# The remainder products of w_out's rest columns on 64 weight columns, and a new order inside the last group

## The reference, cut to what matters

```
h = x @ w_in                             # 192 -> 2048
g = h * (1.0 / (1.0 + np.exp(-1.702 * h)))
return (g @ w_out).astype(np.float32)    # 2048 -> 192
```

## Time and profile before

| what | value |
|---|---|
| median of three runs | 1128.98 us |
| time of the profiled execution | 1129.01 us |
| its span, first to last instruction | 1127.2 us |
| TensorE matmul busy | 1113.8 us (99%) |
| TensorE weight load busy | 914.3 us (81%) |
| VectorE busy | 803.6 us (71%) |
| ScalarE busy | 620.5 us (55%) |
| GpSimd busy | 7.9 us (1%) |

### The profile page before, as it was taken

How to read it: one execution, slowest core, us unless ns; L and a number is a source line. 1 busy time by engine, 2 the same in 40 slices (tenths; PEclk the granted TensorE clock), 3 DMA queues, 4 the chain that set the end, 5 groups by cost and what they waited for, 6 DMA issues and landing times.

```text
span 1127.2 us, 21689 instructions
## 1 busy us (share of the span) xinstructions
PE 1113.8 (99%) x9748; PEld 914.3 (81%) x9748; DVE 803.6 (71%) x714; ACT 620.5 (55%) x655; POOL 7.9 (1%) x9
## 2 busy tenths in 40 slices
PE   7999999999999999999999999999999999999998
PEld 4788878888888888888888888888888888888886
DVE  7998988677576866759667596775867757686322
ACT  6676655565554646455464555545556555454543
POOL 2000000000000000000000000000000000000000
PEclk9999999999999999999999999999999999999999
DMA  8601010101001010010100101001010100100000
GB/s 274 218 7 53 15 53 2 39 29 40 29 1 40 29 40 29 1 40 29 40 29 1 65 4 40 29 22 46 1 40 29 40 29 1 40 29 1 29 1 29
DMA packets 8892, 42.68 MB, mean 38 GB/s; under 512 B 1056, under 2 KB 1312, under 8 KB 6496
## 3 DMA queue, kind: packets, MB, share of 16 engines
q1 hardware_dynamic: 8400, 40.51, 10.9%
q0 software_dynamic: 400, 0.79, 0.4%
HBM read 24.77 MB, written 12.58 MB: 33 GB/s over the span
## 4 chain that ended last, share of the span: by engine, by line
PE 94%; DVE 4%; ACT 1%; DMA 0%; issue 0%; ACTq 0%; DVEq 0%; SPq 0%
PE hid L630 45%; PE acc_main L646 30%; PE acc_rest L646 20%; DVE conv L393 1%; DVE gate_lo L548 1%; DVE prod L386 1%; DMA gate<-in_x_first 0%; ACT gate_hi L313 0%; ACT gate L310 0%; DVE hid L469 0%; DVE w L441 0%; DVE prod L411 0%; DVE prod L463 0%; ACT L255 0%; ACT L310 0%
## 5 line engine op out<-in xcount | busy, mean ns | idle before, releaser
L310 ACT ACTIVATE gate<-hid 128x1024 f32<-128x1024 f32 x256 | 263.1, 1028 | 464.6 <-PE hid L630 463.9
L548 DVE TENSOR_TENSOR gate_lo<-gate,gate_hi 128x1024 fp32r<-128x1024 f32 x256 | 311.5, 1221 | 258.0 <-ACT gate_hi L313 258.0
L630 PE MATMUL hid<-xt,w_hi 64*128 64x512 f32 x3072 | 431.8, 387 | 0.0
L630 PEld LDWEIGHTS hid<-xt,w_hi 64*128 64x128 f32 x3072 | 287.4, 184 | 62.7 <-ACT gate_hi L313 2.1
L646 PE MATMUL acc_main<-gate_hi,w 64*128 64x512 f32 x2048 | 315.8, 386 | 0.7 <-DVE gate_lo L548 0.7
L313 ACT ACTIVATE gate_hi<-hid 128x1024 fp32r<-128x1024 f32 x256 | 261.1, 1020 | 0.0
L646 PEld LDWEIGHTS acc_main<-gate_hi,w 64*128 64x128 f32 x2048 | 191.5, 184 | 42.0 <-DVE gate_lo L548 1.7
L630 PE MATMUL hid<-xt,w_lo 64*128 64x512 f32 x1536 | 215.8, 386 | 0.0
L646 PE MATMUL acc_main<-gate_lo,w 64*128 64x512 f32 x1024 | 199.4, 386 | 0.0
L646 PE MATMUL acc_rest<-gate_hi,w 64*128 64x512 f32 x1024 | 199.4, 386 | 0.0
L646 PE MATMUL acc_rest<-gate_lo,w 64*128 64x512 f32 x1024 | 199.4, 386 | 0.0
(11 more groups left out here) (54 smaller groups left out, 228.1 us busy)
## 6 DMA issues: line engine op xcount, KB each, us to landing
xwin<-in_x_runs SPq DMA_DIRECT2D x15, 1056.0 KB, 4.9
out<-outs_main SPq DMA_DIRECT2D x13, 512.0 KB, 2.6
out<-outs_rest SPq DMA_DIRECT2D x13, 256.0 KB, 2.9
taps<-in_tap_runs SPq DMA_DIRECT2D x1, 3136.0 KB, 10.0
taps<-in_w_rows SPq DMA_DIRECT2D x2, 1536.0 KB, 9.8
w_hi<-w_hi SPq DMA_DIRECT2D x2, 768.0 KB, 9.5
w_lo<-w_lo SPq DMA_DIRECT2D x2, 768.0 KB, 7.2
out<-outs_main SPq DMA_DIRECT2D x6, 256.0 KB, 2.1
```

The source lines that it names most:

```text
L310: nc.scalar.activation(gate[:, v % 2, :, :], hid[:, v % 2, :, :], ACT.Gelu_apprx_sigmoid).then_inc(gate_ready, 1)
L548: nc.vector.tensor_tensor(gate_lo[:, v % SLOTS, :, :], gate[:, v % 2, :, :], gate_hi[:, v % SLOTS, :, :], ALU.subtract).then_inc(gate_lo_r ...
L630: last = nc.tensor.matmul(hid[:, v % 2, h, :], w[rows, k if j else slice_of(h, k), q, f], xt[rows, j % 2, part, k, :], start=(i == 0), sto ...
```

## The change

The helper `halves` gets an argument for the output partitions. Both pairs that multiply `gate_lo` with the rest columns now take `REST_HI` (64 weight columns) in place of `REST_COLS` (128) and write partitions 0 to 63 of `acc_rest` alone. The product of the gates' remainders with the weights' remainders is thereby not computed. In the straight group on `acc_rest` the `gate_lo` pair now precedes the `gate_hi` pair, which carries `stop` and the increment of `rest_added`; in the crosswise group the order stays, since the `gate_hi` pair carries `start`.

```diff
-                def halves(acc, g, cols, crossed, start, stop):
+                def halves(acc, g, cols, crossed, start, stop, out=slice(0, P)):
...
-                        done = nc.tensor.matmul(acc[:, h, :], w2[rows, chunk[h], cols], g[rows, s, h, :],
+                        done = nc.tensor.matmul(acc[out, h, :], w2[rows, chunk[h], cols], g[rows, s, h, :],
...
                 halves(acc_rest, gate_hi, REST_COLS, True, first, False)
-                halves(acc_rest, gate_lo, REST_COLS, True, False, False).then_inc(rest_crosswise, 1)
+                halves(acc_rest, gate_lo, REST_HI, True, False, False, LOWER).then_inc(rest_crosswise, 1)
                 wait(pe, main_straight, n + 1)
                 halves(acc_main, gate_hi, MAIN, True, False, False)
                 halves(acc_main, gate_hi, MAIN_LO, True, False, False)
                 halves(acc_main, gate_lo, MAIN, True, False, last_unit).then_inc(main_added, 1)
                 wait(pe, rest_crosswise, n + 1)
-                halves(acc_rest, gate_hi, REST_COLS, False, False, False)
-                halves(acc_rest, gate_lo, REST_COLS, False, False, last_unit).then_inc(rest_added, 1)
+                halves(acc_rest, gate_lo, REST_HI, False, False, False, LOWER)
+                halves(acc_rest, gate_hi, REST_COLS, False, False, last_unit).then_inc(rest_added, 1)
```

## The result

The changed kernel takes 1138.32 us (median of four runs, 1138.18 to 1138.72) against 1129.07 us (four runs, 1128.92 to 1129.29): ratio 1.0082, 95% interval 1.0065 to 1.0100. It is slower, as forecast, by 9.25 us and not by 177. The forecast of 1306 us and its range from 1145 us are both missed; the loss is a twentieth of the size predicted.

What follows compares the result with a forecast made beforehand. TensorE's stream, filling 99% of the span, was taken as the bound. The profiled 1129.0 us plus 177 us from (b), with nothing from (a), (c) and (d), gave 1306 us; range 1145 to 1405 us.

Steps and rivals of the forecast that it cites:

- (d): Precision and other engines: the dropped product costs no instruction; ScalarE and VectorE only wait longer, with no stall of theirs.
- (a): Number of instructions in the two narrowed pairs: none added or removed, only a hidden load is halved; worth nothing.
- below nothing: Floor of (a): if the pair's 0.013 us above its columns' time went with the width, 6.8 us gained, 1122.2 us.
- Rival C: Width sits in the pair's step: two of 19 pairs a unit save 3.4 to 6.8 us, 1125.6 to 1122.2 us; chance 0.07.
- (b): Shape of the tile: four changes a unit around narrow pairs each drain the array and expose a load; 177 us in all.
- D: Drain at a change of tile shape: the new load waits 0.09 us beyond the last old matmul's slot.
- Rival B: A narrow pair is nothing new to the array, only the weight-column count falls: no change, 1129 us; chance 0.13.
- (c): New order of the straight group: still four shape changes a unit, no wait added; worth nothing.

Runs made afterwards that it cites:

- narrow_all: Kernel before with 64 weight columns in all pairs of both products, except the first two units' first product and each piece's first and last second product: 1143.09 us.
- rows128: Kernel before with the four half-row gate_lo matmuls on the rest columns replaced by two on all 128 rows, and two waits moved earlier: 1281.82 us.
- cross_only: Changed kernel with only the crosswise gate_lo pair narrow; the straight one is wide again and still first of its group: 1133.70 us.
- cols112: Changed kernel with 112 weight columns in place of 64 in the two gate_lo pairs of acc_rest: 1133.80 us.
- half_r0: Kernel before with 64 weight columns in only the first matmul (rows 0 to 63) of the crosswise gate_lo pair, its partner keeping 128: 1134.11 us.
- cols96: Changed kernel with 96 weight columns in place of 64 in the two narrow pairs of a unit, writing partitions 0 to 95: 1141.66 us.
- short_510: Kernel before with 510 moving columns in place of 512 in the crosswise gate_lo pair, all loads 128 wide: 1138.30 us.
- order_only: Kernel before with only the new order of the straight group on acc_rest, 128 weight columns everywhere: 1129.00 us.
- rows_all: Kernel before with the second product as ten matmuls on all 128 rows in place of ten pairs of half-row ones: 1244.79 us.

## Why the prediction was wrong

**What bounds the kernel** and that everything on TensorE's stream counts one for one: right. Other engines only waited a little longer, as (d) said. Two of its readings are loose and change nothing: the 0.33 us between the transposes' starts are three steps and not four, and the 0.7 us is what the second product's matmuls waited, while its weight loads waited 1.7 us.

**(a) No gain from fewer weight columns**: right in sign and in its main reason. No pair of 64 columns steps faster than 226.7 ns for long; narrow_all, with all pairs narrow, averages 229.8. Rival C is refuted. What (a) missed is that fewer weight columns, though their load is hidden, can cost: the 9.25 us belong here, not to (b), and my floor "below nothing" looked only for a gain.

**(b) The drain at each change of shape: the step that failed.** It put D = 0.09 us and an exposed load at each of four changes of columns a unit, 0.69 us. Its price was right for a change of rows and its object wrong. A change in the number of rows costs 0.20 us, as read at the one place of the trace, and rows128 confirms it in the stream. But a change in the number of columns, which the edit makes, costs none of it: the loads of narrow and wide pairs start within 5 ns of each other's matmuls, none is exposed, and the unit grew by 0.040 us in place of 0.69. No run exposes a 64-column load, so its 0.055 us stay unmeasured. The forecast named the step from rows to columns as its weak point and gave the case "no drain" 0.20 in all, rivals B and C; that case is what the chip does. cross_only, cols112 and half_r0 give one and the same figure of steps with 64 or 112 columns, in both or one matmul of a pair, cols96 loses more than 64 columns do, and short_510 loses 9.2 us with no change of tile, so the 9.25 us don't go by the shape. The Trainium skill, TensorEngine Tiling (Array Packing), Key Properties, says that a change of tiling mode drains TensorE. The runs agree where 64 rows become 128 and back, 0.20 us each in rows128, and show nothing held back where 128 weight columns become 64 and back. Whether a pair with 64 weight columns is another mode to the array at all they don't tell: the trace gives only the number of columns.

**(c) The new order** costs nothing: right, order_only.

**Rival B** (no drain, 1129 us) had the mechanism but for the 0.8% that no rival held: the upset of the beat. The figure could be seen in the trace of before, in the steps of 236, 229, 232 and 231 ns behind the head's stalls, if the starts had been read in nanoseconds. That two such figures could come in each unit was not thought of.

**What is shown and what stays open.** Shown: a single matmul with 64 weight columns (half_r0), or a pair whose stream is two columns shorter (short_510), puts the pairs behind it off their beat for four to ten steps; with 120 columns it is one step; the order changes nothing, and a row half left out costs no time. Open: why. That it is the load and not the narrower output that acts is likely, since the narrow pair's own start has already moved (225.9 ns in the changed kernel, 233.3 with 120 columns), but no run separates the two. The loss does not rise steadily with the columns left out, and 127 columns are free. That the loads and the streams contend for something that admits them in steps of 6.67 ns would fit the multiples, but no run here shows what it is.

No version came out ahead of the kernel before. Neither the 128-row matmuls nor the narrow ones gained pace, and the even beat of equal pairs with 128 weight columns is the best that was seen.

## What to carry to other kernels

Read a cost where it was paid and ask which property was changed there: the trace had one costly change of tile, in rows, and the edit changed columns. Trimming weight columns or a few moving columns can cost time in a stream that keeps TensorE full, whether what is trimmed was hidden or paid for: here equal pairs with 128 weight and 512 moving columns kept a beat of 226.7 ns, and one odd instruction broke it for up to ten steps. When such a kernel loses under 1% with no new wait in the profile, take the starts in nanoseconds and average each position of the loop.

## What the runs showed of the hardware that was not expected

- Two moving columns fewer in one pair of 19 cost 9.2 us in 1129; eight fewer cost 10.95 us.
- A weight load's record is 184, 183, 178, 171, 158, 132 and 104 ns for 128, 127, 120, 112, 96, 64 and 32 columns, some 0.83 ns a column on a constant of 77 ns.
- Single 128-row matmuls of type fp32r with 512 moving columns step by 224 to 236 ns in a row of ten (rows_all), no faster on average than pairs of 64-row ones at 226.7, and a change between the two costs 0.20 us.
- One narrow matmul in one row half (half_r0) leaves the two halves 16.7 ns apart in place of 3.3, and the figure runs through both, in the partner one step later.
- The unit's extra length came in multiples of 6.67 ns in all kernels whose feed-forward matmuls all take 64 rows and whose steps were read, but for narrow_all.
